# Gated-attention prologue: three chunks write x's layout in PSUM by products with padded weights, and SyncE stores the result in a loop over tiles

## The reference

```
state = alpha[t][:, None] * state + outer(k[t], v[t])        # per batch and head
y[t]  = q[t] @ state                                         # attention output
x = y in (token, H*D) layout                                 # 3072 x 384
x = (sigmoid(x @ w_gate) * (x @ w_val)) @ w_out              # 384 -> 1536 -> 384
h = max(max(x @ w1, x @ w2), x @ w3)                         # 384 -> 768
out = h @ w_out2                                             # 3072 x 384
```

## Time and profile before

| what | value |
|---|---|
| median of 3 runs | 844.16 us (844.14 to 844.74) |
| the profiled execution's own time | 844.45 us |
| its span, first to last instruction | 842.7 us |
| PE busy | 833.3 us, 99% of the span, 6667 rows |
| DVE, ACT, POOL busy | 384.7, 274.8, 74.5 us |
| TensorE clock granted | 1.00 in every slice |

### The profile page before, as it was taken

The page is one execution under the profiler, slowest core; times in us unless marked ns, Lnnn a source line. Parts: engine busy times, 40 slices in busy tenths (PEclk is TensorE's granted clock), DMA queues, the critical chain, the costliest instruction groups (busy, mean ns, idle before and its releaser), DMA issues.

```text
span 842.7 us, 15954 instructions
## 1 busy us (share of the span) xinstructions
PE 833.3 (99%) x6667; PEld 730.4 (87%) x6667; DVE 384.7 (46%) x932; ACT 274.8 (33%) x490; POOL 74.5 (9%) x68
## 2 busy tenths in 40 slices
PE   8999999999999999999999999999999999999998
PEld 7899999999999988788878888888888888888886
DVE  8787555556567656554653322323223232332321
ACT  4655333333333333334333333312212122221312
POOL 1000111111111101110210043100000000000000
PEclk9999999999999999999999999999999999999999
DMA  7441111111112211110112022000101001010101
GB/s 289 168 179 49 54 49 48 55 49 49 54 49 84 69 46 38 60 57 13 41 45 85 1 75 75 1 1 1 38 0 37 0 0 37 0 37 0 38 0 39
DMA packets 14271, 42.35 MB, mean 50 GB/s; under 512 B 1888, under 2 KB 5472, under 8 KB 14208
## 3 DMA queue, kind: packets, MB, share of 16 engines
q1 hardware_dynamic: 14144, 41.41, 14.0%
q10 hardware_dynamic: 64, 0.05, 0.0%
HBM read 35.56 MB, written 4.72 MB: 48 GB/s over the span
## 4 chain that ended last, share of the span: by engine, by line
PE 96%; DVE 2%; DMA 1%; issue 0%; ACT 0%; SPq 0%; DVEq 0%
PE ps_gv L1041 35%; PE ps_out L1065 19%; PE ps_gv L1047 18%; PE ps_out L1157 6%; PE ps_sc L1041 6%; PE ps_sc L1047 3%; PE ps_pair L1157 2%; PE ps_pair L1014 1%; PE ps_pair L995 1%; PE ps_pair L946 1%; PE ps_sc L966 1%; PE ps_sc L980 1%; PE ps_pair L966 0%; DVE rdec L714 0%; DVE decay L699 0%
## 5 line engine op out<-in xcount | busy, mean ns | idle before, releaser
L1041 PE MATMUL ps_gv<-x_hi,w_hi 128*128 128x512 f32 (+1 forms) x720 | 267.2, 371 | 1.4 <-ACT x_hi L473 1.4
L1041 PE MATMUL ps_gv<-x_hi,w_lo 128*128 128x512 f32 (+1 forms) x720 | 264.7, 368 | 0.0
L1047 PE MATMUL ps_gv<-x_lo,w_hi 128*128 128x512 f32 (+1 forms) x720 | 226.2, 368 | 0.0
L1041 PEld LDWEIGHTS ps_gv<-x_hi,w_hi 128*128 128x128 f32 x720 | 135.2, 188 | 17.7 <-issue 1.5
L1047 PEld LDWEIGHTS ps_gv<-x_lo,w_hi 128*128 128x128 f32 x720 | 133.8, 188 | 17.9
L1041 PEld LDWEIGHTS ps_gv<-x_hi,w_lo 128*128 128x128 f32 x720 | 135.3, 188 | 15.7
L813 DVE TENSOR_TENSOR h_sb<-act_sb,ps_gv 128x384 f32<-128x384 f32 (+1 forms) x84 | 51.2, 610 | 149.2 <-PE ps_gv L1047 149.2
L473 ACT ACTIVATE h_hi<-h_sb 128x384 fp32r<-128x384 f32 (+1 forms) x84 | 48.0, 571 | 146.5 <-DVE h_sb L813 146.1
L517 ACT ACTIVATE act_sb<-ps_gv 128x384 f32<-128x384 f32 (+1 forms) x84 | 45.1, 537 | 141.2 <-PE ps_gv L1047 141.2
L910 DVE TENSOR_TENSOR probs<-probs,ps_gv 128x512 f32<-128x512 f32 x36 | 24.7, 687 | 138.4 <-PE ps_gv L1047 138.4
L777 DVE TENSOR_TENSOR h_lo<-h_sb,h_hi 128x384 fp32r<-128x384 f32 (+1 forms) x84 | 51.7, 615 | 49.1 <-ACT h_hi L473 49.1
(11 more groups left out here) (128 smaller groups left out, 969.6 us busy)
## 6 DMA issues: line engine op xcount, KB each, us to landing
inbuf<-att_in SPq DMA_DIRECT2D x23, 704.0 KB, 4.5
mid<-w SPq DMA_DIRECT2D x12, 576.0 KB, 7.5
inbuf<-att_in SPq DMA_DIRECT2D x23, 256.0 KB, 2.8
inbuf<-w SPq DMA_DIRECT2D x6, 768.0 KB, 4.4
out<-inbuf SPq DMA_DIRECT2D x5, 768.0 KB, 3.5
out<-inbuf SPq DMA_DIRECT2D x4, 192.0 KB, 2.5
mid<-att_in SPq DMA_DIRECT2D x1, 704.0 KB, 8.9
x_raw<-x_raw SPq DMA_DIRECT2D x18, 32.0 KB, 1.9
```

Of the source, the lines that this page charges most:

```text
L1041: mm(bank, w_at(half, f, c + k * P, total=total), x_hi[:, k, 0:w], start=(k == 0 and half == 0), stop=False)
L1047: return mm(bank, w_at(0, f, c + k * P, total=total), x_lo[:, k, 0:w], start=False, stop=(k == KT - 1))
```

## The change

The diff does four things.

1. For chunks 0 to 2, y's products write x's own layout: `x_bank(C)`, three slices of 128 rows in one PSUM bank. The fourth pair of heads is written by products whose weights are padded: a 64-column block that is zero but for 16 columns (`v_pad`, `state_pad`, in the memory of `x_raw`, zeroed and filled by POOL). So `attend(C)` is replaced by `values_first(C)` (12 products) and `states_first(C)` (12 products, for chunks 1 and 2), in that order, with a wait on `y_first` inside. ACT rounds x straight from PSUM (`x_first`) and DVE makes the rest from PSUM (`x_first_rest`). The copies to `x_raw`, the six transfers of tile 0, and the whole-tile `x_split` and `x_rest` of tile 0 are gone.
2. The numbers of `unused` products are 5 and 1 where they were 10 and 9.
3. The table of steps has a row of its own for tile 0, with the backward scan and the scaling of q and k as entries of their own.
4. SP's stores are one loop over six tiles with four stores each.

```diff
-THREE = {"scan": (0, 3, 6), "score": (2, 5, 8), "add": (4, 7, 9)}
+START_UP = {"scan": (-1, 3, 5), "recip": (1, 4, 6), "scale": (2, 5, 7), "score": (3, 6, 8), "add": ()}
+THREE = {"scan": (0, 3, 6), "recip": (0, 3, 6), "scale": (), "score": (2, 5, 8), "add": (4, 7, 9)}
-STEPS = (THREE, THREE, THREE, FOUR, FOUR, FOUR)
+STEPS = (START_UP, THREE, THREE, FOUR, FOUR, FOUR)
...
 SP
-            move_last(0, (0, 2))
...
-            for T in range(TILES2 - 1):
-                sp.wait_ge(o_evac, T * SUB + SUB)
-                sp.dma_start(out[T], stage_out).then_inc(stored, 16)
-            for s in range(SUB):
-                sp.wait_ge(o_evac, (TILES2 - 1) * SUB + s + 1)
-                sp.dma_start(out[TILES2 - 1][:, s, :], stage_out[:, s, :]).then_inc(stored, 16)
+            with sp.Fori(0, TILES2) as T:
+                for s in range(SUB):
+                    sp.wait_ge(o_evac, T * SUB + s + 1)
+                    sp.dma_start(out[T][:, s, :], stage_out[:, s, :]).then_inc(stored, 16)
...
 POOL
+            def pad_state(C):
+                pool.wait_ge(state_done, C)
+                for r in range(2):
+                    p, n = head_at(r, KT)
+                    ins = nc.gpsimd.tensor_copy(last_parts(state_pad(C), r),
+                                                state[:, state_at(C, 0), p, :].rearrange("p (k c) -> p k c", k=KT))
+                ins.then_inc(state_padded, 1)
...
+            pad_v(0)
+            pad_v(1)
+            pad_state(1)
+            pad_v(2)
             pool.wait_ge(kh_done, 2 * PRO)
             split_first(0).then_inc(w_lo_part, 1)
             split_first(1).then_inc(w_lo_part, 1)
+            pad_state(2)
             split_first(2).then_inc(w_lo_done, 1)
...
 ACT
+            def x_first(C):
+                act.wait_ge(y_done, C + 1)
+                copy(x_hi[:, :, C * CH:(C + 1) * CH], x_bank(C)).then_inc(x_hi_done, 1)
...
             khs_copy(2)
             violation(1)
-            y_copy(1)
-            y_copy(2)
...
+            x_first(1)
             split_w1(2)
+            x_first(2)
...
 DVE
+            def x_first_rest(C):
+                dve.wait_ge(x_hi_done, C + 1)
+                t = slice(C * CH, (C + 1) * CH)
+                nc.vector.tensor_tensor(x_lo[:, :, t], x_bank(C), x_hi[:, :, t].bitcast(F32),
+                                        ALU.subtract).then_inc(x_lo_done, 1)
...
 PE
+            def states_first(C):
+                pe.wait_ge(mask_done, 2 * C)
+                pe.wait_ge(state_padded, C)
+                for r, half in enumerate(HALVES):
+                    p, n = head_at(r, KT)
+                    for k in range(KT):
+                        mm(x_bank(C)[r * ODD:(r + 1) * ODD, k, :], state_pad(C)[HALVES[n], r, k * ODD:(k + 1) * ODD],
+                           att(buf(C), Q, HALVES[n])[:, p, :], start=(k == 0), stop=False, skip_group_check=True)
+                for k in (2, 0, 1):
+                    if k == 0:
+                        pe.wait_ge(y_first, C)
+                    for r, half in enumerate(HALVES):
...
+            def values_first(C):
+                pe.wait_ge(v_padded, C + 1)
                 pe.wait_ge(mask_done, 2 * C + 2)
...
             scores(1)
             transposes(1)
-            attend(0)
+            values_first(0)
             outer(1)
-            unused(10, ident, ident)
+            states_first(1)
+            unused(5, ident, ident)
             scores(2)
             transposes(2)
-            attend(1)
-            attend(2)
+            values_first(1)
+            states_first(2)
+            values_first(2)
             outer(2)
-            unused(9, ident, ident)
+            unused(1, ident, ident)
```

More of the change, by code:

```diff
@@ L801, in layer1 @@
                     g = T * NF1 + f
-                    scanned, scored, added = (chunk_at(T, f, steps) for steps in ("scan", "score", "add"))
-                    if scanned == PRO:
-                        scanned = None
+                    scanned, scored, added = (chunk_at(T, f, what) for what in ("scan", "score", "add"))
+                    inverted, scaled = chunk_at(T, f, "recip"), chunk_at(T, f, "scale")
                     if scanned is not None:
@@ L1016, in attend @@
                                start=(p < 2 and s == (1 if first else 0)), stop=False, skip_group_check=True)
[L1017 to L1031 removed]
+                for p in range(PAIRS):
+                    for n in range(2):
+                        ins = value(C, p, n, n)
@@ new lines, in attend @@
+                if not crossed(C):
+                    ins.then_inc(y_same, 1)
+                    pe.wait_ge(y_same, C + 1 - PRO)
+                for p in range(PAIRS):
+                    for n in range(2):
+                        ins = value(C, p, n, 1 - n, start=crossed(C))
+                ins.then_inc(y_done, 1)
+            def states_first(C):
+                pe.wait_ge(mask_done, 2 * C)
+                pe.wait_ge(state_padded, C)
+                for r, half in enumerate(HALVES):
+                    p, n = head_at(r, KT)
+                    for k in range(KT):
+                        mm(x_bank(C)[r * ODD:(r + 1) * ODD, k, :], state_pad(C)[HALVES[n], r, k * ODD:(k + 1) * ODD],
[4 more added lines that the diff above has]
+                    for r, half in enumerate(HALVES):
+                        p, n = head_at(r, k)
+                        ins = mm(x_bank(C)[half, k, :], state[HALVES[n], state_at(C, 0), p, :],
+                                 att(buf(C), Q, HALVES[n])[:, p, :], start=False, stop=False, skip_group_check=True)
+                    if k == 2:
+                        ins.then_inc(y_first, 1)
@@ new lines, in values_first @@
+            def values_first(C):
+                pe.wait_ge(v_padded, C + 1)
+                pe.wait_ge(mask_done, 2 * C + 2)
+                for r, half in enumerate(HALVES):
+                    p, n = head_at(r, KT)
+                    for k in range(KT):
+                        mm(x_bank(C)[r * ODD:(r + 1) * ODD, k, :], v_pad(C)[:, r, k * ODD:(k + 1) * ODD],
+                           probs_of(C)[:, PAIRS * n + p, :], start=(C == 0 and k == 0), stop=False, skip_group_check=True)
+                for r, half in enumerate(HALVES):
+                    for k in range(KT):
+                        p, n = head_at(r, k)
+                        ins = mm(x_bank(C)[half, k, :], v_cols(buf(C), (2 * p + n) * D, D),
+                                 probs_of(C)[:, PAIRS * n + p, :], start=False, stop=True, skip_group_check=True)
```

134 lines of the change are left out of this document (59 added, 75 removed).

## The result

The changed kernel takes 846.01 us, the median of 17 executions (845.29 to 846.25); the kernel before took 844.28 in the same comparison (843.98 to 845.12, 17 executions). The ratio is 1.0019, with a 95% interval of 1.0013 to 1.0026. So it is 1.73 us slower where I had forecast 1.15 us faster, 0.4 us above the upper end of the range (845.6).

What follows compares the result with a forecast made beforehand. PE was taken to bound the kernel after the start. Prologue -2.05, tile 0 +1.20 and stores -0.30 gave -1.15 us against a median of 844.16: 843.0 us, range 841.8 to 845.6.

Steps and rivals of the forecast that it cites:

- The pace of the new products: Prologue output products: each array part has its own queue, 0.11 us a pass; 0.44 us dearer per V, 1.13 per S.
- V: A chunk's 12 output products with v in the prologue (V0 is chunk 0's): 1.45 us predicted, 1.01 before.
- S: A chunk's output products with the state in the prologue (S1 is chunk 1's): 1.72 us predicted, 0.59 before.
- value product 0: Block 0's value product, from which PE runs without a hole: predicted to move from 29.24 to 27.19, -2.05 us.
- The prediction's own sign: A first layer-1 product after 27 us, or no PE wait in blocks 3 to 6, makes the prediction wrong.
- The first rival: Padded output products run one behind the other: 0.65 us more per V, 0.44 per S, 2.8 in all, 845.85; chance 0.17.
- scores 2: Chunk 2's scores in the prologue: predicted start 18.65 us, where they started at 18.35, so +0.30.
- At about the same time: Prologue: outer(2) and one unused product end about when gate product 0 starts, at 25.55 us.
- The lost cover of the unused products: Prologue: ten unused products were hidden by PE's wait for DVE; new work uses that cover up, +0.30 us.
- POOL's padding: Filling chunk 2's state padding: ready at 21.1 us, before S at 21.72; the rival that it is late: 843.8, chance 0.12.
- Tile 0: New table makes PE wait for k scaling, the mask behind outer 3, and chunk 4's k: +0.40, +0.60, +0.20, sum +1.20 us.
- The stores: Last stores at the end: up to 0.8 us back without a slow issue, +0.3 with one; middle taken, -0.3 us.

Runs made afterwards that it cites:

- the halves in turn: Changed kernel with the loops over half and column group exchanged, so output products alternate between halves of the array; 844.70 us, ratio to before 1.0003.
- the six in a row: Changed kernel with each V written half by half, six products to half 0 and then six to half 1; 847.98 us in one execution.
- The run with one product: Changed kernel with halves in turn and scores one block later, plus one unused product for five ahead of chunk 2's scores; 842.83 us, ratio to before 0.9985.
- the run with the old steps: Changed kernel with tile 0's table of steps as before the change, chunk 3's backward scan ahead of layer 1; 845.87 us, ratio to before 1.0017.

## Why the prediction was wrong

**The pace of the new products, the step that failed.** The prediction said "So each part has its own queue and a product need not wait for one ahead of it that goes to another part. I carry this over to the new order, in which three products in a row go to the same half." The rows it rested on, 0,1,1,0, never have more than two products (four passes) in a row for one part, which is the most that costs next to nothing. Three in a row start the other half 0.27 us late, in each of V0, S1, V1, S2 and V2: value product 0 is at 28.99 in the changed kernel and at 27.69 with the halves in turn, 1.30 us. That is 1.30 of the 1.80 us by which the prologue missed. The prediction's own sign came true as well: the first layer-1 product starts at 27.33, after 27. With turns, V, S and the time to x_first(2) (23.73 to 25.30) are 1.46, 1.73 and 1.57, for the predicted 1.45, 1.72 and 1.57. The first rival had the mechanism by halves: it priced no passing at all, 0.65 and 0.44 us, where the measured cost is 0.27. That its time, 845.85, lies close to the measured 846.01 is luck: it counted 2.8 us for what measured 1.30, and the rest is the 0.50 below, the stores' -0.30 that did not come and an end that is usually longer. The rule of strict order that the prediction cites from the Trainium skill ("TensorE: Matmul & The Clock Gate", Part 3, "The mechanism") does not agree with the row at 21.74, nor with the six in a row, where the other half starts three passes before the first half is through.

**The rest of the prologue.** The remaining 0.50 us are in the run with turns: scores 2 at 18.91 for 18.65, which is 0.10 from what stands ahead and 0.16 from a longer changeover behind the unused products (17.60 to 18.91, counted as 1.15); and gate product 0 at 26.05, of which the other 0.24 arise there: the unused product behind outer(2) ends at 26.04, while ACT's copy (25.30, 0.49) had ended at 25.79. "At about the same time" was 0.25 us too kind.

**The lost cover of the unused products** was rightly named ("the new work uses the cover up"), and worth more than said: +1.06 for the predicted +0.30, of which 0.50 is the pace of V0 and S1, counted above. The run with one product took back 0.53 by cutting it to what DVE allows.

**POOL's padding** was not late: 20.59 to 20.97, with S of chunk 2 at 22.76 (predicted 21.1 and 21.72).

```profile
20.59 0.38 POOL L478 COPY x_raw<-state 128x48 f32<-128x48 f32 x2 [0.28 <-DVE state L777]
```

**Tile 0** was right in place, cause and size: 0.41, 0.65 and 0.27 for 0.40, 0.60 and 0.20. That DVE's state update and forward scan had been free in PE's stall, and that the old table would lose as much without it, was not seen; the run with the old steps showed it.

**The stores**, -0.30 taken from two ends far apart, show no effect by median. In the profiled pair the end is 0.12 us shorter (3.75 for 3.87). The long issue took 0.56 to 1.15 us in ten executions with the loop and 1.33 and 1.41 in the two with written-out stores, but the medians show no gain from it.

**The sum.** For the profiled pair: -0.25 + 1.33 is 1.08, of which 0.97 is left at the last product (where the other 0.11 went stays open), and the end gives back 0.12. That is 0.85, measured 0.84. The medians differ by 0.9 us more. 0.72 of it is that the profiled execution of the changed kernel was its shortest, 0.17 that the one of before was above its median. In the execution with the written-out stores, which is 0.64 us longer than the profiled one, 0.55 of that lay behind the last product (4.30 for 3.75). Why the end is usually longer with the new products stays open: in all of them an instruction transfer runs beside the last stores, but it does so in the kernel before too, and moving or merging the stores did not win it back.

## What to carry to other kernels

When small products use only a part of the array, write them so that the parts take turns; two in a row for one part cost next to nothing, three in each of two halves cost 0.27 us a group here, six 0.93. When a stall on the critical path is removed, list what the other engines did during it: here 2.2 us of DVE's work (a state update and a scan) had been free, and without the stall PE lost 1.2 to 1.3 us under two tables, until the scores were moved one block later. And read a price from a row only as far as its pattern goes: a rule that holds for two in a row is not shown for three.

## What the hardware showed unexpectedly

- In these orders a pass starts once the pass four places ahead of it in the program has started, if its own part of the array is free: 21.306 behind 21.300 with three products in a row, 22.67 with the ninth pass with six in a row, almost none with two (V 1.50 for 1.46) or with turns.
- A store's issue on SyncE can be long until an instruction transfer (q8, 16 KB, 0.88 to 1.45 us) has ended. In 12 profiled executions one issue began 0.14 to 0.72 us after the transfer's start and ended 0.27 to 0.46 us after its end, in ten of them 0.36 to 0.39. It lasted 0.56 to 1.41 us where its neighbours take 0.33 to 0.45. With two stores per tile it began 1.02 us after the start and ended 0.47 us after the end. Meeting the transfer is not enough: in seven of these executions an issue that began 0.00 to 0.14 us after its start took the usual 0.33 us and ended while it ran.
- The one store that was issued from ACT's queue in the same place had an issue of 0.38 us, though an instruction transfer ran beside it (837.47 to 838.35, issue at 837.72), and landed after 3.4 us, against a median of 2.3 for SyncE's three beside it and 2.4 in the changed kernel.
